# Repeating the pooled attention rows into x by SBUF-to-SBUF transfers instead of by matmuls, behind the first batch

## The reference

```python
out_d = sm_attn(q_d, k_d, v_d)             # q, k, v averaged over groups of 4 rows: 144 pooled rows
out_up = np.repeat(out_d, factor, axis=2)  # each pooled row stands 4 times: 576 rows
scores = np.where(mask, scores, -1e9)      # mask: |pos - pos'| < 4
out_local = np.matmul(attn, v)             # attention of each row to its 7 neighbours
x = out_up + out_local                     # heads side by side: 576 x 512
mixed = np.real(fft(fft(x, axis=1), axis=2)); u = x + mixed
y = u + np.maximum(norm(u) @ w_ch1, 0) @ w_ch2
out = (sigmoid(causal_conv5(y)) * (y @ w_val)) @ w_out
```

## Time and profile before

| | |
|---|---|
| median of 3 runs | 778.94 us (778.38 to 779.45) |
| the profiled execution, its own time | 778.96 us |
| its span (first to last instruction) | 777.2 us |
| mean granted TensorE clock | 0.978 |
| TensorE busy | 710.3 us (91% of the span) |
| VectorE, ScalarE, GpSimd busy | 388.1, 193.1, 152.6 us (50%, 25%, 20%) |

### The profile page before, as it was taken

One profiled execution on the slowest core, in us unless ns is written; L12 is line 12 of the kernel. 1 busy time (PEld: TensorE's weight loads), 2 busy tenths in 40 slices (PEclk: granted clock), 3 DMA queues, 4 the chain that ended last, 5 costly groups with the idle time before them and its releaser, 6 DMA issues.

```text
span 777.2 us, 15619 instructions
## 1 busy us (share of the span) xinstructions
PE 710.3 (91%) x5960; PEld 535.3 (69%) x5960; DVE 388.1 (50%) x925; ACT 193.1 (25%) x417; POOL 152.6 (20%) x131
## 2 busy tenths in 40 slices
PE   2567849999999998999999998999999999999998
PEld 1444536877777776777777776877777677777776
DVE  4446585554554872543553871543553861123452
ACT  1535522322212122222212132222212131111201
POOL 8001577991101311000201311000201200000000
PEclk9999768999999999999999999999999999999999
DMA  9994138122000127022001027022000000000001
GB/s 261 291 250 108 31 139 191 23 62 67 11 1 32 39 81 184 3 58 63 18 1 31 31 81 192 2 51 69 18 1 1 1 32 31 1 1 1 2 18 43
DMA packets 42246, 49.00 MB, mean 63 GB/s; under 512 B 4803, under 2 KB 35846, under 8 KB 41094
## 3 DMA queue, kind: packets, MB, share of 16 engines
q1 hardware_dynamic: 32608, 31.06, 15.9%
q10 hardware_dynamic: 9574, 16.99, 7.1%
HBM read 43.32 MB, written 4.72 MB: 62 GB/s over the span
## 4 chain that ended last, share of the span: by engine, by line
PE 78%; DVE 6%; SPq 5%; DMA 4%; POOL 3%; issue 2%; ACT 1%; ACTq 0%; POOLq 0%; DVEq 0%
PE P L563 24%; PE Y L580 23%; PE P L696 4%; PE Y L685 4%; PE Y L696 3%; PE A L592 3%; PE P L685 3%; SPq L429 2%; SPq L433 2%; PE A L550 2%; PE A L543 2%; PE A L533 2%; PE A L635 1%; DMA kl<-qk_win 1%; PE A L646 1%
## 5 line engine op out<-in xcount | busy, mean ns | idle before, releaser
L563 PE MATMUL P<-unT,w_wv 128*128 128x288 f16 x1536 | 211.6, 289 | 5.7 <-issue 4.8
L580 PE MATMUL Y<-hT,w 128*128 128x288 f16 x1536 | 215.1, 286 | 0.0
L563 PEld LDWEIGHTS P<-unT,w_wv 128*128 128x128 f16 x1536 | 149.9, 99 | 50.7 <-issue 11.7
L1144 DVE SCALAR_TENSOR_TENSOR hT<-P,hT 128x288 f16<-128x288 f32 x128 | 58.5, 457 | 252.2 <-ACT hT L820 252.1
L580 PEld LDWEIGHTS Y<-hT,w 128*128 128x128 f16 x1536 | 145.7, 98 | 42.2 <-issue 5.9
L820 ACT ACTIVATE hT<-P 128x288 f16<-128x288 f32 x128 | 52.4, 410 | 216.1 <-PE P L563 215.6
L1180 DVE SCALAR_TENSOR_TENSOR gate<-xT,cw,gate 128x288 f32<-128x288 f32 x128 | 68.5, 535 | 4.5
L791 ACT ACTIVATE prob_or_un<-prob_or_un 73x288 f32<-73x288 f32 (+1 forms) x52 | 23.3, 448 | 93.1 <-DVE prob_or_un L1017 89.2
L1315 POOL MEMSET x<- 1x512 f32 x4 | 2.1, 516 | 213.7 <-ACT x L809 213.7
L319 POOL TENSOR_TENSOR x<-x,fb 128x256 f32<-128x256 f32 (+1 forms) x12 | 12.1, 1007 | 105.5 <-DVE fb L1085 105.5
L696 PE MATMUL P<-shared,wo 128*128 128x288 f32 x128 | 32.1, 409 | 0.7 <-DVE shared L1190 0.5
(11 more groups left out here) (167 smaller groups left out, 833.3 us busy)
## 6 DMA issues: line engine op xcount, KB each, us to landing
kl<-qk_win SPq DMA_DIRECT2D x38, 140.0 KB, 6.9
ql<-qk_win SPq DMA_DIRECT2D x19, 256.0 KB, 6.5
vl<-v_win SPq DMA_DIRECT2D x72, 65.0 KB
pair_or_folded<-qk_pool SPq DMA_DIRECT2D x8, 580.0 KB, 5.9
pair_or_spectrum<-qk_pool SPq DMA_DIRECT2D x8, 580.0 KB, 7.3
out<-ot ACTq DMA_DIRECT2D x32, 144.0 KB, 1.8
w_wv<-w_ch ACTq DMA_DIRECT2D x4, 1024.0 KB, 12.0
w<-w_ch ACTq DMA_DIRECT2D x4, 1024.0 KB, 11.1
```

Of the source, the lines that this page charges most:

```text
L563: last = mm(P[s % 2][:, 0:HN], w1s(k, f, wt), unT[:, ut, k, ha * HN:(ha + 1) * HN], start=k == 0 and wt + ut == 0, stop=k == KD - 1 and wt ...
L580: last = mm(Y[d][:, 0:HN], w2s(f, d, wt), hT[s % 3][:, ht, :], start=f == 0 and wt + ht == 0, stop=f == KF - 1 and wt == 1)
L1144: nc.vector.scalar_tensor_tensor(out=hT[s % 3][:, 1, :], in0=P[s % 2][:, 0:HN], scalar=0.0, in1=hT[s % 3][:, 0, :], op0=ALU.max, op1=ALU.s ...
```

## The change

For the first batch nothing changes. In the three rounds of the loop TensorE no longer does the L543 matmuls, and the small matmuls write with start=True. The pooled rows are written into `x` by transfers from `xd` that ScalarE issues at slots 10 to 14, one tile a slot (`repeat_pooled`, `REPEAT_AT`), split as `pooled_rows` lists: (first row, end row, tile, half, first pooled row, number of pooled rows). ScalarE's copy `unit_out` is dropped there, and VectorE adds the local rows in PSUM to the rows in `x` (`unit_add`), waiting for both.

```diff
+        ld_up = [sem(f"ld_up{t}") for t in range(NT)]
...
+        REPEAT_AT = 10
...
+        def pooled_rows(t):
+            if t < 2:
+                return [(0, 128, t, 0, 32 * t, 32)]
+            if t == 2:
+                return [(1, 125, 3, 1, 0, 31), (125, 128, 3, 1, 31, 1)]
+            if t == 3:
+                return [(0, 1, 4, 1, 31, 1), (1, 125, 4, 1, 32, 31), (125, 128, 4, 1, 63, 1)]
+            return [(0, 32, 2, 0, 64, 8), (32, 33, 2, 0, 72, 1), (0, 1, 5, 1, 63, 1), (1, 29, 5, 1, 64, 7), (29, 32, 5, 1, 71, 1)]
...
                     t = u - UD
-                    if t == 0:
-                        pe.wait_ge(normed, UD * (b + 1))
-                        if not later(b):
+                    if opening(b):
+                        if t == 0:
+                            pe.wait_ge(normed, UD)
                             pe.wait_ge(spread_made, 2)
...
-                                      V[:, w // 2 + 2 * (w % 2), :, i, 0:D], start=False, stop=True, skip_group_check=True)
+                                      V[:, w // 2 + 2 * (w % 2), :, i, 0:D], start=not opening(b), stop=True, skip_group_check=True)
...
+            def repeat_pooled(b, t):
+                if t == 0:
+                    act.wait_ge(normed, UD * (b + 1))
+                    act.sem_inc(passed, 1)
+                for lo, hi, tile, rev, first, groups in pooled_rows(t):
+                    src = xd[first:first + groups, rev, :].unsqueeze(1).to_broadcast([groups, (hi - lo) // groups, DM])
+                    act.dma_start(x[lo:hi, tile, :], src).then_inc(ld_up[t], 16)
...
                     for u in unit_at(b, m, s, LAG_AV):
-                        if u >= UD:
+                        if u >= UD and m is None:
                             unit_out(b, u)
+                    if b is not None and m is not None and 0 <= s - REPEAT_AT < NT:
+                        repeat_pooled(b, s - REPEAT_AT)
...
+            def unit_add(b, u):
+                t = u - UD
+                dve.wait_ge(av_done, b * NU + u + 1)
+                dve.wait_ge(ld_up[t], 16 * len(pooled_rows(t)) * b)
+                R = banks(b, u)[2]
+                for tile, lo in [(LOCAL_TILE[t], 0)] if t < 4 else [(2, 0), (5, 2 * LQ)]:
+                    r = XROWS[tile]
+                    last = tt(x[0:r, tile, :], R[lo:lo + r, :], x[0:r, tile, :], ALU.add)
+                last.then_inc(x_sb, 1)
...
                         if m is not None:
+                            for u in unit_at(b, m, s, LAG_AV):
+                                unit_add(b, u)
```

More of the change, by code:

```diff
@@ L536, in unit_av @@
                     t = u - UD
-                    if t == 0:
-                        pe.wait_ge(normed, UD * (b + 1))
-                        if not later(b):
+                    if opening(b):
+                        if t == 0:
+                            pe.wait_ge(normed, UD)
                             pe.wait_ge(spread_made, 2)
[L541 to L544, removed]
+                        for tile, lo, r in ([(LOCAL_TILE[t], 0, 128)] if t < 4 else [(2, 0, 2 * LQ), (5, 2 * LQ, 2 * LQ)]):
+                            first = 128 * (tile % 3) + (1 if tile < 3 else 0)
+                            mm(R[lo:lo + r, :], spread[:, first:first + r], xd[:, tile // 3, :], start=True, stop=False, skip_group_check=True)
                         pe.wait_ge(probT_done, n + 1)
@@ L804, in unit_out @@
                 act.wait_ge(av_done, b * NU + u + 1)
-                if t == 0 and later(b):
-                    act.wait_ge(uT_ps, 6 * b)
                 R = banks(b, u)[2]
```

## The result

The changed kernel takes **801.72 us** (median of 4 runs, 800.77 to 802.65), the kernel before 778.66 us (4 runs, 778.1 to 779.45): a ratio of **1.0314**, 95% interval 1.0288 to 1.034. It is 23 us slower. The forecast was 795 us, within 778 to 811, slower with 80%.

What follows compares the result with a forecast made beforehand. TensorE, busy 91% of the span, was taken as the bound. Per round -4.45 saved, +7.7 stall, +0.3 issues, +1.8 clock make +5.35 us; three rounds +16.0 on 778.96 give 795 us, range 778 to 811.

Steps and rivals of the forecast that it cites:

- TensorE is the bound, 13.35 us are taken away: In the change's slots TensorE is always busy; dropping the repeating matmuls saves 4.45 us a round, 13.35 in three.
- The issues by themselves are free: ScalarE's twelve transfer issues a round, 0.34 to 0.61 us each by nearest rows, fit in slack and cost nothing.
- One engine for 124 rows: Each transfer of 31 pooled rows four times (tiles 3 and 4) puts all 124 pieces of 2 KB on one engine.
- The rival of the spread transfers: Long transfers go on several engines or the queue takes them all; ScalarE is never held: 765.6 us, 11%.
- 90 ns a piece: One engine moves a 2 KB piece of a long transfer in 90 ns, so 124 pieces take 11.2 us.
- So I put the limit at about 125 pieces an engine: ScalarE's issue of the second long transfer, slot 13, waits for the first to drain, retiring at 184.0 us, not 172.3.
- A stall of 7.7 us and 0.3: Each round TensorE waits 7.7 us in slot 15 for `probT`; slot 14's five issues delay unit 10 by 0.3.
- 1.8 us of clock: Behind the stall TensorE's granted clock falls, costing 1.8 us a round, bounds 0 to 3.7.
- The sum: Per round -4.45 + 7.7 + 0.3 + 1.8 = +5.35 us; three rounds +16.0, giving 795 us.
- held not, but late: ScalarE goes on, but the second long transfer or q and k loads land late for TensorE: 771.6 us, 6%.
- gain and loss cancel: The queue holds more, the hold ends at about 180.5, the clock stays, stall 4.2 us: 778 us, 4%.
- Window loads starve too: SyncE's issues are held by the same full engine; values or q and k come 3 to 6 us late: 812 to 825, 7%.

Runs made afterwards that it cites:

- e3: The changed kernel without its transfers and without VectorE's wait for them: 763.14 us, ratio 0.9803 to the kernel before.
- e1: The changed kernel with both 124-row transfers cut into 64 and 60 rows, spread over 16 and 15 engines: 763.96 us, ratio 0.982 to the kernel before.
- e8: The changed kernel with each 124-row transfer cut into 68 rows (17 pooled rows) and 56 rows (14 pooled rows): 767.84 us, ratio 0.9917 to before.
- e10: e1's kernel with seven groups of repeating transfers issued by ScalarE behind its last store, to time the hold: 848.21 us, a single run.
- e11: The changed kernel with the two 124-row transfers issued by SyncE behind q and k loads instead of by ScalarE: 791.19 us, ratio 1.0205 to before.
- e6: The changed kernel with the three rows behind each 124-row transfer issued ahead of it: 797.14 us, ratio 1.0291 to the kernel before.
- e7: The changed kernel with only the second 124-row transfer (t = 3, slot 13) cut into 64 and 60 rows: 778.8 us, ratio 1.0066 to before.
- e2: The changed kernel with only the first 124-row transfer (t = 2, slot 12) cut into 64 and 60 rows: 769.27 us, ratio 0.9887 to before.

## Why the prediction was right where it was, and where not

- **TensorE is the bound, 13.35 us are taken away**: shown by e3 (14.4 us, by its interval 10 to 20) and e1.
- **VectorE's additions cost nothing**: 685 ns each, and e1 and e3 have TensorE without a gap.
- **The issues by themselves are free**: yes in e1 (0.58 to 1.05 us each). The row of a strided load on SyncE (0.61) was the nearer one; the store's 0.34 is not reached.
- **One engine for 124 rows**: shown by the marks (one each), by e8 for 17 pooled rows, by e10's 25 GB/s. The rival of the spread transfers ends here, and its price (765.6) is near what e1 measures when they are spread on purpose (763.96). The rule of the Trainium skill (DMA: Bandwidth & Descriptors, section "Why a DMA increments its semaphore by 16 and not by 1"), which spreads a transfer by the largest number up to 16 that divides both sides, is what these counts show.
- **90 ns a piece**: in e10, with nothing else under way, 81; in the changed kernel, by its packet records, 95 for the first long transfer (168.66 to 180.48 us) and 102 for the second (180.77 to 193.40), with SyncE's loads under way. The forecast added 1.8 us for these loads, which makes 104 ns of its 90.
- **"So I put the limit at about 125 pieces an engine. The first long transfer [...] just fits. The second does not fit until the first has drained"**: this step failed. The limit is some 90 pieces of 2 KB, and it doesn't hold the transfer that goes over it but an issue behind. (Of the pieces counted for the earlier trace rows 96 were of 512 or 560 B, and for small ones e10 finds 111 to 113; the number was carried over to 2 KB.) So the first long transfer brings a hold too (4.83 us), and the large one begins behind the second and ends when that one is down to its last 93 pieces, not when the first is gone. Counted from the end of `probT` of unit 8 (169.93 us before, 167.38 after), the forecast had the first long transfer gone, and the hold over, after 14.1 us, SyncE's loads included. It was gone after 13.1, and the hold went on until 16.9 (184.26), while 31 pieces of the second moved.
- **A stall of 7.7 us and 0.3**: it was 9.81 and 0.83. On the same count TensorE, without the 0.83, would have stood ready after 9.3 us (187.31 - 9.81 - 0.83 = 176.67) where the forecast had 9.1, and from the end of the hold to TensorE it took 3.05 us for 2.75. So of the 2.9 us by which the two gaps exceed 7.7, 2.8 are the hold's and 0.3 the chain's behind it, less 0.2. The 0.83 in slot 14 come from the first hold, not, as forecast, from the issues of slot 14.
- **1.8 us of clock**: 2.0, 3.1 and 3.3. The row of a 2.1 us gap was a fair guess for the first round and low for the others; the bound of 3.7 held. Low by 1 us a round, it is the smaller miss.
- **The sum** was +5.35 us a round, measured +7.7: gaps 2.5 more, clock 1.0 more, saved 0.35 more, and 0.8 the other way of which 0.3 are the transposing's. The path was right (one engine, ScalarE's issuing held, the `relu` late, TensorE waiting for `probT` in slot 15), and the size of the hold is the term that was too small. That it was no further off is in part luck: by the forecast's rule for the end of a hold, at the speed that the pieces had, it would have ended 3.8 us sooner than it did.
- **Rivals**: "held not, but late" and "gain and loss cancel" did not come. "Window loads starve too" is not in the changed kernel, where TensorE waits for no landing of vl in these slots; it came when e11 moved the transfers to the loads' queue.

## What to carry to other kernels

Count, for each transfer inside SBUF, into how many equal shares (up to 16; the 17 rows of e8 went on one engine) both sides divide. Where that is one, every piece goes through one engine, here at 25 GB/s or less, and the engine that issues is held at one of the next issues until some 90 pieces of 2 KB are left. Cut such a transfer into parts that divide (16 and 15 groups for 31): two more issues a round, of 0.6 to 1.05 us each, turned +23 us into -14. A queue's issuer should have nothing behind it that a tight chain needs. Moving the same transfer to another queue only moves the hold to what stands there, and in e11 the loads behind it had to wait for its pieces as well.

## What the runs showed of the hardware that was not expected

- The issue that goes over the limit retires in 0.7 to 1.4 us (2.61 once, in e11); one behind it is held, whatever its size (in e6 a single row for 4.06 us by its record, 32 rows for 7.78).
- Behind a long transfer short issues take mostly 1.0 to 1.7 us each for several issues (e7: 5.31 for four, 3.06 in e1), on SyncE's queue too: its eight value loads took 9.45 us in the changed kernel, 7.03 before.
- The limit is 86 to 94 pieces of 2 KB but 111 to 113 of 1 KB or 512 B (e10).
- What is issued behind a long transfer on its own queue is moved behind it on that engine (e11: the value pieces of that engine begin at 188.31, those of the others were in by 187.46).
- In the first round of e2 the issue behind the long transfer was not held (three issues of slot 13 in 2.12 us), in the two other rounds it was, for 4 us; in the third of e6 and e7 it was the second issue behind. What differs was not found.
